# A gated linear recurrence laid out by feature, with decays over groups of four tokens

## What is computed

```python
def _attn_ref(r, k, v, w, u) -> np.ndarray:
...
    for t in range(S):
...
        cur = np.einsum('bhd,bhe->bhde', u[None] * kt, vt)
        y[:, :, t] = np.einsum('bhd,bhde->bhe', rt, state + cur)
        state = wt[:, :, :, None] * state + np.einsum('bhd,bhe->bhde', kt, vt)
```

## Time and profile before

| | us |
|---|---|
| median of three runs | 836.35 (830.28 to 843.3) |
| profiled execution, span | 833.9 |
| recurrence: start of the run to the next stage's first transfer | 267.5 |
| TensorE busy in the span | 692.3 |
| VectorE, ScalarE, GpSimd busy | 538.6, 381.8, 219.2 |

### The profile page before, as it was taken

How to read it: one execution, slowest core, us unless ns; L and a number is a source line. 1 busy time by engine, 2 the same in 40 slices (tenths; PEclk the granted TensorE clock), 3 DMA queues, 4 the chain that set the end, 5 groups by cost and what they waited for, 6 DMA issues and landing times. The chain is left out here.

```text
span 833.9 us, 13780 instructions
## 1 busy us (share of the span) xinstructions
PE 692.3 (83%) x4453; PEld 638.2 (77%) x4453; DVE 538.6 (65%) x1069; ACT 381.8 (46%) x912; POOL 219.2 (26%) x237
## 2 busy tenths in 40 slices
PE   2568878877894699999999955898979897889887
PEld 2568778877884699999999955776967695779666
DVE  5697897788511667656666633687378647854884
ACT  1121222122212646657566534577357635753673
POOL 7174577476742000000000003013102400240021
PEclk9998889797956799999999986999989999999999
DMA  9776658867451500300301012740363055206321
GB/s 151 142 129 148 126 139 180 152 117 148 113 181 68 151 1 1 114 1 0 113 0 57 1 43 79 180 98 1 105 166 72 11 132 142 57 31 139 65 48 57
DMA packets 138401, 76.33 MB, mean 92 GB/s; under 512 B 113500, under 2 KB 127220, under 8 KB 138356
## 3 DMA queue, kind: packets, MB, share of 16 engines
q1 hardware_dynamic: 138356, 75.77, 39.3%
HBM read 33.25 MB, written 14.16 MB: 57 GB/s over the span
## 5 line engine op out<-in xcount | busy, mean ns | idle before, releaser
L1077 POOL TENSOR_TENSOR att_o_lo<-att_o_t,att_o_hi 64x256 fp32r<-64x256 f32 x48 | 37.6, 783 | 261.9 <-ACT att_o_hi L1156 261.5
L568 PE MATMUL rec_ps<-rec_r_p,rec_k_bd 96*128 96x128 f32 x384 | 64.0, 336 | 37.5 <-DMA rec_r_p<-rec_rt 23.9
L568 PEld LDWEIGHTS rec_ps<-rec_r_p,rec_k_bd 96*128 96x128 f32 x384 | 60.0, 246 | 39.2 <-issue 37.2
L1351 PE MATMUL att_ps<-att_ident,att_a 128*128 128x128 f32 x336 | 60.1, 290 | 24.2 <-DVE att_a L1254 19.6
L1132 ACT ACTIVATE att_a<-att_ps,att_nmax 128x128 f32<-128x128 f32 (+2 forms) x96 | 60.8, 633 | 37.0 <-DVE att_nmax L1239 36.6
L62 PE MATMUL hid_ps<-hid_g_lo,hid_w_hi 128*128 128x384 f32 x192 | 67.2, 350 | 6.3 <-DVE hid_g_lo L822 6.2
L62 PE MATMUL hid_ps<-hid_x_lo,hid_w_hi 128*128 128x384 f32 x192 | 66.7, 347 | 6.6 <-ACT hid_conv_sb L785 5.8
L509 DVE TENSOR_TENSOR rec_a_t<-rec_ps,rec_later 128x512 f32<-128x512 f32 x48 | 32.8, 688 | 53.6 <-PE rec_ps L568 52.9
L812 DVE SCALAR_TENSOR_TENSOR hid_cv<-hid_h,hid_conv_sb,hid_cv 128x768 f32<-128x768 f32 x64 | 65.0, 1015 | 2.9 <-ACT hid_cv L745 1.8
L1351 PEld LDWEIGHTS att_ps<-att_ident,att_a 128*128 128x128 f32 x336 | 37.4, 144 | 38.1 <-ACT att_at_hi L1145 13.3
L64 PE MATMUL hid_ps<-hid_g_hi,hid_w_hi 128*128 128x384 f32 x192 | 66.2, 345 | 0.0
(11 more groups left out here) (151 smaller groups left out, 1982.3 us busy)
## 6 DMA issues: line engine op xcount, KB each, us to landing
att_qq_hi<-att_q_hi SPq DMA_DIRECT2D x32, 192.0 KB, 3.7
att_qq_lo<-att_q_lo SPq DMA_DIRECT2D x32, 192.0 KB, 4.0
rec_w_nat<-in_w SPq DMA_DIRECT2D x24, 192.0 KB, 3.8
rec_k_nat<-in_k SPq DMA_DIRECT2D x24, 192.0 KB, 4.5
rec_r_nat<-in_r SPq DMA_DIRECT2D x24, 192.0 KB, 4.6
rec_v_nat<-in_v SPq DMA_DIRECT2D x24, 192.0 KB, 3.9
x_features<-rec_x_t SPq DMA_DIRECT2D x8, 576.0 KB, 4.3
hid_x_t<-x_features SPq DMA_DIRECT2D x12, 384.0 KB, 5.4
```

What stands on the lines that cost most here:

```text
L568: m = mm(bank[3 + half][:, P * q:P * (q + 1)], k_bd[:, n, odd, P * c:P * (c + 1)], r_p[:, n, P * c:P * (c + 1)], start=True, stop=True)
L1077: G.tensor_tensor(o_lo[rows, ep, cols], o_t[rows, ep, cols], o_hi[rows, ep, cols].bitcast(F32), ALU.subtract).then_inc(o_lo_ready, 1)
L1351: m = nc.tensor.transpose(bank[TB[q % 3]][:, P * (j - lo):P * (j - lo + 1)], a[:, t % NA, P * j:P * (j + 1)], ident[:])
```

## The change

The host hands the inputs over already laid out: w, k and r by feature (one contiguous 4.6 KB row a partition and half batch), v by chunk, u as a block diagonal. The transposes of w, k and r are gone. Odd heads lie on partitions 64 to 111 and even heads on 0 to 47, so a score matmul has K = 48. The decays are multiplied up over groups of four tokens (products of two, then of four, then a scan of 153 elements for all nine feature tiles and chunks of the half batch at once, in each direction). Inside a group GpSimd and VectorE multiply k and r by what is missing. The bonus becomes three small matmuls, ScalarE writes it as a scaled identity into the score tile `a_t`, and VectorE copies the scores over it where the mask holds (`copy_predicated`). The output comes by feature (v is the weights, 64 columns, the score tile streams in 128), so `turn_y` is gone too. The state is added and scaled on VectorE (`advance`). All chunks are written out, without a loop. The moves of g and of r have ten pieces now, as those of k.

```diff
-            def load(b, h, arrays):
-                for x, dst, loaded in arrays:
-                    for c in range(CH * h, CH * h + CH):
-                        sp.dma_start(dst[:, c, :].rearrange("p (h d) -> p h d", h=H),
-                                     x[one(b), :, P * c:P * (c + 1), :].rearrange("b h p d -> p (b h) d")
-                                     ).then_inc(loaded[h], 16)
...
-            def move_r(b, h):
-                half = slice(HALF * h, HALF * (h + 1))
-                for lo, hi in pieces(F, D2):
...
-                    sp.dma_start(r_p[lo % D2:lo % D2 + hi - lo, lo // D2, half],
-                                 rt[lo % P:lo % P + hi - lo, lo // P, half]).then_inc(moved_r[h], 16)
+            def load_wkr(hb):
+                n, s2, s3 = hb // 2, hb % 2, hb % NKR
+                if hb >= 2:
+                    sp.wait_ge(turned_in, 2 * (hb - 1))
+                    sp.wait_ge(p2_ready, hb - 1)
+                sp.dma_start(w_f[:, s2], w_img[hb]).then_inc(ld_w[s2], 16)
...
+                sp.dma_start(k_f[:, s3], k_img[hb]).then_inc(ld_k[s3], 16)
+                sp.dma_start(r_f[:, s3], r_img[hb]).then_inc(ld_r[s3], 16)
+            def load_v(hb):
+                if hb >= 2:
+                    sp.wait_ge(y_psum, CH * (hb - 2) + CH)
+                sp.dma_start(v_n[:, hb % 2, 0:CH * F], v_img[hb]).then_inc(ld_v[hb % 2], 16)
+            def move_g(hb):
...
+                if b > 0:
+                    sp.wait_ge(st_ready, step(C * (b - 1) + (CH - 1 if h == 0 else C - 1)))
+                sp.wait_ge(g_ready, hb + 1)
+                for lo, hi in rows:
+                    at = 64 * (lo // D % 2) + lo % D
+                    sp.dma_start(g_p[at:at + hi - lo, lo // D // 2, cs],
                                  g_f[lo % P:lo % P + hi - lo, lo // P, cs]).then_inc(moved_g[h], 16)
...
+            def move(hb, dst, src, ready, moved):
+                if hb >= 2:
+                    sp.wait_ge(a_psum, 2 * (CH * (hb - 2) + CH))
+                    if dst is r_p:
+                        sp.wait_ge(y_psum, CH * (hb - 2) + CH)
+                sp.wait_ge(ready, 2 * hb + 2)
+                for lo, hi in rows:
+                    at = 64 * (lo // D % 2) + lo % D
+                    sp.dma_start(dst[at:at + hi - lo, hb % 2, lo // D // 2, :],
+                                 src[lo % P:lo % P + hi - lo, hb % NKR, lo // P, :]).then_inc(moved[hb % 2], 16)
+            def store(hb):
+                b, h = divmod(hb, 2)
+                sp.wait_ge(y_taken, CH * hb + CH)
+                for odd in range(2):
+                    sp.dma_start(x_dram[b, :, HT * h:HT * (h + 1)].rearrange("(n o d) s -> o d n s", o=2, d=D)[odd],
+                                 x_p[64 * odd:64 * odd + D, hb % 2]).then_inc(x_stored[hb % 2], 16)
+            load_wkr(0)
+            sp.dma_start(u_bd[:], u_img).then_inc(s_u, 16)
+            for hb in range(NB):
+                if hb + 1 < NB:
+                    load_wkr(hb + 1)
+                load_v(hb)
+                if hb == 3:
                     load_next(sp)
...
+                move_g(hb)
+                if hb >= 2:
+                    store(hb - 2)
+                move(hb, k_p, k_f, k_ready, moved_k)
+                move(hb, r_p, r_f, r_ready, moved_r)
+            store(NB - 2)
+            store(NB - 1)
...
-            def multiply(b, c):
...
-                G.tensor_tensor(rk[:], r_nat[:, c, :], k_nat[:, c, :], ALU.mult).then_inc(rk_ready, 1)
-                wait(pool, bonus_ready, C * (b - 1) + c + 1)
-                wait(pool, rk_ready, C * b + c + 1)
-                G.tensor_tensor(rku[:, c, :], rk[:], u_all[:], ALU.mult).then_inc(rku_ready, 1)
...
+            for hb in range(NB):
+                s2, s3 = hb % 2, hb % NKR
...
+                G.tensor_tensor(rk[:, s2], r_f[:, s3], k_f[:, s3], ALU.mult).then_inc(rk_ready, 1)
+                pool.wait_ge(rk_ready, hb + 1)
+                pool.wait_ge(ld_w[s2], 16 * (hb // 2 + 1))
+                k2, r2, w2 = pairs(k_f[:, s3]), pairs(r_f[:, s3]), pairs(w_f[:, s2])
+                G.tensor_tensor(k2[:, :, 0], k2[:, :, 0], w2[:, :, 1], ALU.mult).then_inc(turned_in, 1)
+                G.tensor_tensor(r2[:, :, 1], r2[:, :, 1], w2[:, :, 0], ALU.mult).then_inc(turned_in, 1)
...
+            def own(i):
+                act.wait_ge(bon_psum, i + 1)
+                A.activation(bon[:, i % 2], bank[6][:, F:F + H], ACT.Copy).then_inc(bon_ready, 1)
+                if i >= NA:
+                    act.wait_ge(y_psum, i - NA + 1)
+                act.wait_ge(bon_ready, i + 1)
+                for h in range(H):
+                    A.activation(a_t[:, i % NA, h % 2, h // 2], ident[:], ACT.Copy,
+                                 scale=bon[:, i % 2, h:h + 1]).then_inc(diag_ready, 1)
...
+            for i in range(LEAD):
+                own(i)
+            copy_ends(0)
+            take_ks(0)
+            copy_ends(1)
...
-            def scan(b, h):
...
-                    V.tensor_tensor_scan(flat(e_up[:, ft, cs]), flat(w_up[:, ft, cs]), flat(restart[:]), 0.0,
-                                         ALU.mult, ALU.add)
-                    V.tensor_tensor_scan(flat(e_lo[:, ft, cs])[:, ::-1], flat(w_lo[:, ft, cs])[:, ::-1],
-                                         flat(restart[:]), 0.0, ALU.mult, ALU.add).then_inc(scanned, 1)
...
+            def products(hb):
+                s2 = hb % 2
+                dve.wait_ge(ld_w[s2], 16 * (hb // 2 + 1))
+                if hb >= 1:
+                    dve.wait_ge(sc_ready, 2 * hb)
+                w2 = w_f[:, s2].rearrange("p t (n two) -> p (t n) two", two=2)
+                V.tensor_tensor(p2[:].rearrange("p g two -> p (g two)"), w2[:, :, 0], w2[:, :, 1],
+                                ALU.mult).then_inc(p2_ready, 1)
+                dve.wait_ge(p2_ready, hb + 1)
+                q = halves(p2[:])
+                V.tensor_tensor(g_lo[:, :, 0:HG], q[:, :, 0, :, 0], q[:, :, 0, :, 1], ALU.mult).then_inc(group_ready, 1)
+                V.tensor_tensor(g_up[:, :, 1:HG + 1], q[:, :, 1, :, 0], q[:, :, 1, :, 1], ALU.mult).then_inc(group_ready, 1)
...
+                dve.wait_ge(group_ready, 2 * hb + 1)
+                V.tensor_tensor_scan(flat(e_lo[:, s2])[:, ::-1], flat(g_lo[:])[:, ::-1], flat(restart[:]), 0.0,
+                                     ALU.mult, ALU.add).then_inc(scanned, 1)
+                dve.wait_ge(group_ready, 2 * hb + 2)
+                V.tensor_tensor_scan(flat(e_up[:, s2]), flat(g_up[:]), flat(restart[:]), 0.0,
+                                     ALU.mult, ALU.add).then_inc(scanned, 1)
+            def scales(hb):
+                b, h, s2 = hb // 2, hb % 2, hb % 2
+                if hb >= 1:
+                    dve.wait_ge(k_ready, 2 * hb)
+                    dve.wait_ge(r_ready, 2 * hb)
+                dve.wait_ge(scanned, 2 * hb + 1)
+                V.reciprocal(r_sc[:, :, 0], e_lo[:, s2, :, 0:HG]).then_inc(inv_ready, 1)
+                dve.wait_ge(scanned, 2 * hb + 2)
+                V.reciprocal(k_sc[:, :, 1], e_up[:, s2, :, 1:HG + 1]).then_inc(inv_ready, 1)
...
+                if h == 0:
+                    V.tensor_tensor(g_f[:, :, 0:CH - 1], up[:, :, 0:CH - 1, HG], lo[:, :, 1:CH, 0], ALU.mult).then_inc(g_ready, 1)
...
+                dve.wait_ge(ends_copied, 2 * hb + 2)
+                dve.wait_ge(inv_ready, 2 * hb + 2)
+                V.tensor_tensor(k_sa[:], k_sc[:].rearrange("p c h g -> p (c h g)"), p2[:, :, 1], ALU.mult).then_inc(sc_ready, 1)
+                V.tensor_tensor(r_sb[:], r_sc[:].rearrange("p c h g -> p (c h g)"), p2[:, :, 0], ALU.mult).then_inc(sc_ready, 1)
...
+                V.tensor_tensor(k4[:, :, 0:2], k4[:, :, 0:2], by(k_sa[:]), ALU.mult).then_inc(k_ready, 1)
+                V.tensor_tensor(k4[:, :, 2:4], k4[:, :, 2:4], by(k_c), ALU.mult).then_inc(k_ready, 1)
+                dve.wait_ge(turned_in, 2 * hb + 2)
+                V.tensor_tensor(r4[:, :, 0:2], r4[:, :, 0:2], by(r_c), ALU.mult).then_inc(r_ready, 1)
+                V.tensor_tensor(r4[:, :, 2:4], r4[:, :, 2:4], by(r_sb[:]), ALU.mult).then_inc(r_ready, 1)
+            def prepare(hb, part):
+                (products, scales, decay)[part](hb)
...
-            def mask(b, c):
-                wait(dve, y_psum, C * b + c - 1)
-                for half in range(2):
-                    wait(dve, a_psum, 2 * (C * b + c) + half + 1)
-                    V.tensor_tensor(a_t[:, c % 2, 512 * half:512 * (half + 1)].rearrange("p (n s) -> p n s", s=P),
-                                    bank[3 + half].rearrange("p (n s) -> p n s", s=P),
-                                    later[:].unsqueeze(1).broadcast_to([P, 4, P]), ALU.mult).then_inc(a_ready, 1)
+            def mask(i):
+                dve.wait_ge(diag_ready, H * i + H)
+                for odd in range(2):
+                    dve.wait_ge(a_psum, 2 * i + odd + 1)
```

(60 more changed lines are left out.)

580 lines of the change are left out of this document (210 added, 370 removed).

## The result

The changed kernel takes 846.2 us in the median of four runs (842.72 to 847.83), the kernel before 833.32 (828.09 to 843.3): a ratio of 1.016, 95% interval 1.011 to 1.022. It is 1.6% slower, inside the 2% that counted as no change, though the interval reaches just past it. The profiled span is 844.3 where the prediction's sum gave 846.1.

What follows compares the result with a forecast made beforehand. SyncE's DMA issues in a closed loop bind: second start 65.1, six periods of 30.6 (8.7 + 21.9) to 248.7, tail 31.0, next stage at 279.7, 12.2 us later than now; from 833.9 that gives 846 us, own range 836 to 858.

Steps and rivals of the forecast that it cites:

- The queue gets no lighter: SyncE's issues per half batch: 35 DMAs become 36, at 0.62 us each 22.3 us.
- rival 2: Clock stays low through the output: v issued at T (half batch's score start) + 12.0, period 33.9, 872 us; chance 0.20.
- The closed loop: Scores, mask, g_f, g moves, stores, k and r moves, next scores; SyncE idles until g_f is there; period 30.6 us.
- The front of the loop: From a half batch's first scores until g_f (8.3 us) and the v load's issue, the later at 8.7 us.
- I take no overlap: TensorE: even and odd heads' matmuls do not run side by side; every pass takes its own 0.107 to 0.113 us.
- rival 1: Heads side by side: scores and output cost half, g_f 6.5 us after the start, period 28.4, 821 us; chance 0.26.
- The rest of the loop: SyncE's g moves 6.2, stores 1.2, k and r moves 12.4 with 0.2 of waits, landing 1.9: 21.9 us.
- The start: Everything before the first half batch's scores: first start at 36.8 us, 4.4 later than 32.38 before.
- at under the 0.23: ScalarE's diagonal copies at the start: 0.17 us each, 1.65 a chunk, 4.9 for three chunks.
- The end: From the last half batch's start to the next stage: 31.0 us, so that stage starts at 279.7.
- Rival 3: Issues get cheap, SBUF moves at 0.33 us each; TensorE binds at 25 us a half batch, 803 us; chance 0.12.
- TensorE idle 5 to 8 us: Sign that the forecast is right: TensorE idles this long before each half batch's start while SyncE issues without a gap.

Runs made afterwards that it cites:

- a_g_twice: The changed kernel with SyncE issuing every g move twice, the copy going to a tile nobody reads: 889.74 us, ratio 1.070 to the kernel before.
- a_g_behind: The changed kernel with SyncE's ten g moves put behind the k and r moves instead of ahead: 828.96 us, ratio 0.995 to the kernel before.
- a_v_three: The changed kernel with three buffers of v, its load issued with w, k and r: 835.71 us, ratio 1.005 to the kernel before.
- a_hid_late: The changed kernel with the next stage's weights (3.1 MB) loaded in half batch 6 instead of 3: 843.1 us in a single execution.
- a_ends_first: The changed kernel with ScalarE's first copies of the scanned ends ahead of its 24 diagonal copies: 838.43 us, ratio 1.009 to the kernel before.

## Why the prediction was right, and where it was not

The time was right to a microsecond, and part of that is luck. By its own steps:

**What bounds.** Right for after: `a_g_twice` priced an added issue at 0.54 us. "The queue gets no lighter" was the core of it: TensorE, VectorE and GpSimd all got lighter, and the kernel did not get faster. For the kernel before, the last start was misread (235.77 for 229.89), so the forecast compared its 30.6 us with 29.1 where 28.2 was true. The sum for the changed kernel does not use that number. The misreading also stands in rival 2: the passes that took 3.29 us lay ten us behind the half batch's start, not four.

**The closed loop.** Right in kind: SyncE idles until v and g_f are there, then issues without a gap up to the next start. `a_g_behind` showed that the place of the g moves alone costs 17 us.

**The front of the loop, forecast 8.7, measured 6.4.** The step that failed is "I take no overlap". Sixteen score passes at the lower level took 2.01 and not 3.57, and the two sets of output passes 3.1 and not 3.53. These were forecast at full clock; the first set still ran at the lower level (132.75 to 134.66, 0.119 a pass against 0.064 at 138.74), so that a later return of the clock ate part of what the overlap gave. TensorE's part came to 6.0 us where 7.7 was taken; the rest of the 2.3 are the allowances for the semaphore and the issue (0.9 taken, 0.5 measured). That is the mechanism of rival 1, which gave g_f at T + 6.5 (6.1 measured). The masks cost 1.35 a pair (1.51 taken), reciprocals 1.05 and 0.99 (1.0), g_f 0.10 (0.53).

**The rest of the loop, forecast 21.9, measured 24.0** (136.34 to 160.31). The mis-sized terms are the g moves, 7.16 for 6.2, and the k moves, 7.59 for 6.2; the r moves took 6.24. The slow ones stand behind the v load and behind the two stores, but not all that stand there are slow: the g moves from 72.51, right behind a v load too, took 6.22. With the g moves last (`a_g_behind`) the k moves took 6.21 and 7.30 in the two half batches from 142.26 on, r and g 6.24 each, and with the weights' loads ahead of them the g moves took 9.4 and 9.6 us. So an issue behind a large transfer often costs more than the median of the earlier trace rows; the maximum there, 1481 ns, hinted at it. What makes it so is not settled: taking v away from in front of g (`a_v_three`) did not bring 6.2 back. 2.3 too much and 2.1 too little are why 30.6 met the 30.4 of this half batch: luck. The mean of 30.76 also holds 0.7 us a period from the weights' loads (34.2 us in one of six), which were priced at nothing.

**The start, forecast 36.8, measured 38.73.** The step that failed is the diagonal copies "at under the 0.23": they took 0.31 each (2.45 for eight), and the three chunks 7.6 us where 4.9 was taken. ScalarE also spent 1.28 us from 12.66 on in an ACT_TABLE_LOAD that the sum left out. More than half of both was hidden because the inputs came sooner than taken (GpSimd's first product ended at 11.0 and not at 13.6). ScalarE reached the ends at 21.60 and not 19.8.

**The end, forecast 31.0, measured 26.2.** Overlap again, but not the 21.2 of rival 1: in the last half batch the lower level held through the first chunk's output, the second chunk's scores and the passes from 262.76 to 264.66, as TensorE's timeline shows.

```profile
253.73 1.98 PE L541 MATMUL rec_ps<-rec_a_t,rec_v_n 128*64 128x128 f32 x16
255.64 1.95 PE L547 MATMUL rec_ps<-rec_r_p,rec_st 48*48 48x128 f32 x16
...
259.92 2.08 PE L488 MATMUL rec_ps<-rec_r_p,rec_k_p 48*128 48x128 f32 x16
```

That it held so long belongs to this execution. In the profiles of `a_hid_late`, `a_v_three`, `a_ends_first` and `a_g_behind` TensorE does the same work behind the last start, the full level is back within the first chunk's output, and the way to the next stage is 22.5 to 22.8 us. So some 3.5 us of what these profiles gain on that of the changed kernel are the clock's and not the edits'.

**The rivals.** Rival 1 is true as a mechanism and false as a time: it took the rest of the loop and the start over unchanged from the forecast. Of rival 2 the clock came in part and the price did not: the first set of output passes behind a start ran at the lower level in the half batch shown, the second at 0.071 a pass from 134.66 on; from 220.73 on the second set was slow too (0.113), and in the last half batch even more. But by the overlap such a set costs 1.9 us and not 3.3, and v was issued 6.0 us behind the start, in that slow half batch 6.7, and never 12. Rival 3 is out: the median issue stayed at 592 ns, and the sentence of the Trainium skill ("DMA: Bandwidth & Descriptors", section "Issuing engines are not separate DMA queues") that initiating a DMA is usually small beside the DMA does not hold for these moves: 0.59 us against a landing of 2.1, ten of them one after the other. The named sign of the forecast, "TensorE idle 5 to 8 us" at a start, was wrong by the overlap: 12.4 to 16.2. Taken by itself it would have spoken for no rival; the distance of the starts decided.

## What to carry to other kernels

Count the DMAs that one queue must issue in a period before counting bytes or flops: here 30 of 36 moved data a few rows sideways, and laying the inputs out so that no move is needed, with more buffers, was worth 84 us, while what the change saved on the engines turned into idle time. Where an issuing queue waits for a result of the very stretch that its transfers start, the whole chain from start to start is the bound, and its order is worth as much as its length. After each gain look for what runs ahead into the freed place: loads that overtook moves took back 15 us here, which one added wait recovered, and an engine that now ran beside another took back more than half of the 8 us won at a start.

## What the runs showed of the hardware

- Two fp32 matmuls on different row groups (K of 48 at partitions 0 and 64) or column groups overlap when they stand next to each other in the program: 0.068 against 0.103 us a score pass, 0.064 against 0.094 for output, at full clock.
- A VectorE operation with both inputs in SBUF stands until the GpSimd operation beside it has ended: 2.90 us for four columns. A mask whose data are in PSUM does not: 1.40 us a pair. The Trainium skill, "SBUF — State Buffer", section "Who interferes with whom", says that a VectorE instruction with two SBUF inputs contends with a GpSimd instruction that reads SBUF, and that the port pair they share is an exclusive lock. The trace agrees. In the changed kernel it made one decay of 0.75 us last 2.22.
- Moves of 24 to 72 KB on ScalarE's queue, beside moves on SyncE's, landed in a median of 2.0 to 2.2 us with no load beside them and in 3.9 to 4.4 with 1.77 MB of loads issued among them.
- copy_predicated on 128x512 from PSUM takes 0.72 us in the mean, 0.04 more than the multiply that it replaced (0.69).
